# Agent attention and two MLPs in one kernel: values moving in column halves, loads reordered, running sums in a PSUM bank, the output scale moved to the end, MLP2 eight places behind

## The chip, the cores and the metric

The kernel runs on one core of a Trainium2 chip. Its time is the device time of one launch in microseconds (us); the median of three runs is the measure. The profile is one further execution. Engines are named as in the profile: PE is TensorE (matmuls; PEld is its weight load), DVE is VectorE, ACT is ScalarE, POOL is GpSimd, and SP is the engine that issues the transfers.

## The reference, cut to what matters

```python
# q, k, v: 12480 x 128; agents: 49 x 128; all float32
def sm(a, b):
    s = (a @ b.T) / sqrt(128)
    e = exp(s - s.max(-1))
    return e / (e.sum(-1) + 1e-9)
agent_v = sm(agents, k) @ v                # 49 x 128, needs every k and v
x = sm(q, agents) @ agent_v                # 12480 x 128
h = x @ w_in1                              # 128 -> 2048
g = where(h >= 1, h, where(h <= -1, 0, (h + 1)**2 / 4))
y = g @ w_out1                             # 2048 -> 128
r = maximum(y @ w_in2, 0)
out = (s * r * r + b) @ w_out2             # s and b are scalars
```

## The kernel before

Start. SP loads the keys in 12 blocks of 1,024 tokens and a rest of 192 (`KV_BLOCKS`), and puts the values block by block into the same slots once the keys there are scored. PE scores keys (`score_k`, L449), ACT copies scores out, and DVE finds maxima. The softmax over all tokens is done in two parts: blocks 0 to 5 (`EARLY`) are shifted by a first maximum, blocks 6 to 12 by the final one. The final one goes through PE twice: `turn_max(1)` (L456) and `spread_max(1)` (L463). DVE shifts a block (`shift_block`, L785), ACT takes the exponentials, DVE sums them (`sum_block`, L790), and PE multiplies values by them (`weigh_v`, L476). In `weigh_v` the 128 x 128 piece of values is the operand that is loaded as weights and the 49 exponentials, given twice (98 columns), are the one that moves. DVE then makes the transposed `agent_v_t` (L838 to L854).

Joined matrix. The kernel never forms x. `make_m` (L514) computes M = agent_v x w_in1 in five parts of 128, 384, 512, 512 and 512 columns; ACT rounds each (`round_m`), DVE makes the rest of it (`split_m`, L858), since all large matmuls run as a high and a low part. So MLP1 of a chunk is probabilities x M.

Chunks. The 12,480 tokens are 25 chunks of `W` = 500. An outer loop `i` takes chunks, an inner loop `j` has 16 places (`TILES`), one for each 128 of the 2,048 inner columns; the number n = 16 i + j is called an item here. At each place PE does, in this order: 2 matmuls of MLP1's first layer for item n (L563, L564), 3 of MLP2's first layer for an item `TILES + MLP2_DELAY` earlier (L582 to L584), 3 of MLP1's second layer for an item some places back (L545 to L547, `multiply_g1`), 3 of MLP2's second layer (L613 to L615). So a full place has 11 matmuls of 500 columns. Of the first chunk only MLP1 exists, and of the last only MLP2: from item 0 until MLP2 begins, a place has 5 matmuls. In the loop `first(i)` is chunk 0.

The first items. For n below `FIRST_ITEMS`, an item passes ACT (`below`, L694), POOL (`square_first`, L990), DVE (L886), ACT (`g1_hi`, L684), DVE (`g1_lo`, `split_g1`, L868), and then PE multiplies it (L545). Its PSUM bank is free for another item when `split_g1` is done (`h1_before`). Items below 16 rotate over five banks, all later ones over three (`h1_bank`). `second_lags` says how many places `multiply_g1` runs behind: 4 in chunk 0, 3 up to item 19, then 2.

Side jobs. Probabilities of chunk c+1 are made during chunk c: `score_q` on PE (L424, place 3), `max_q`, `shift_q`, `sum_q`, `invert_q`, `scale_q` on DVE, `exp_q` on ACT, `round_probs` and `split_probs` on POOL, `turn_probs` on PE (L432, place 12), `keep_probs` on ACT. The bias b x w_out2 summed over its rows is made by `sum_w_out2` (L526): two matmuls with one moving column at each of the places 8 to 15 of chunk 0. POOL multiplies w_out2 by s (L996) and splits it (L975, L977).

The order is the order in which each engine's code is written; engines wait for each other on semaphores. Transfers go through one queue, SP's, in program order.

## Time and profile before

| | |
|---|---|
| three runs | 1104.99, 1103.66, 1103.97 us; median 1103.97 |
| profiled execution, its own time | 1106.1 us |
| its span, first to last instruction | 1104.3 us |
| PE busy | 1088.3 us, 99% of the span |
| ACT, DVE, POOL busy | 924.3, 916.0, 843.7 us |
| PE's granted clock, mean | 0.995 of full |
| bytes read from HBM | 23.40 MB |

The page's chain that ended last is 94% PE and 3% DMA. Busy shares are means over stages that differ: in the first 47 us transfers run without a break, from 96 us on PE does. The views to look at are the tables of stretches and the order of time in the first 96 us.

### The profile page before, as it was taken

How to read it: one execution, taken by the hardware profiler on the slowest of the kernel's cores; microseconds unless marked ns; L12 is line 12 of the kernel's file. 1: busy time of each engine (PE TensorE's matmuls, PEld its weight loads, DVE VectorE, ACT ScalarE, POOL GpSimd, SP SyncE). 2: the span in 40 equal slices, each digit the busy share in tenths (PEclk: the TensorE clock that was granted, in tenths of full speed). 3: DMA queues.
4: the chain of work that ended last, by engine and by line, in shares of the span. 5: the costliest groups of instructions: out<-in, count | busy, mean ns of one | idle time of the engine just before them, and what ended most of it. 6: DMA issues, size and time to landing. Idle time of an engine off the chain costs nothing.

```text
span 1104.3 us, 16796 instructions
## 1 busy us (share of the span) xinstructions
PE 1088.3 (99%) x5349; PEld 911.3 (83%) x5349; DVE 916.0 (83%) x1456; ACT 924.3 (84%) x1745; POOL 843.7 (76%) x1231
## 2 busy tenths in 40 slices
PE   8999999999999999999999999999999999999998
PEld 7877888888888888888888888888888888888886
DVE  4677888888888888889888888888888888888876
ACT  3276888888888888888888888888888888888887
POOL 3565788788788788788788788788788788788760
PEclk9998999999999999999999999999999999999999
DMA  9700000000000000000000000000000000000000
GB/s 367 289 1 1 1 19 20 1 20 19 1 20 19 1 19 20 1 20 19 1 19 20 1 20 19 1 19 19 6 14 19 11 10 19 10 10 11 10 1 19
DMA packets 11864, 30.86 MB, mean 28 GB/s; under 512 B 1568, under 2 KB 8192, under 8 KB 11264
## 3 DMA queue, kind: packets, MB, share of 16 engines
q1 hardware_dynamic: 11776, 29.79, 7.7%
q8 instruction: 42, 0.69, 0.3%
q14 instruction: 46, 0.38, 0.1%
HBM read 23.40 MB, written 6.39 MB: 27 GB/s over the span
## 4 chain that ended last, share of the span: by engine, by line
PE 94%; DMA 3%; DVE 1%; ACT 1%; issue 0%; SPq 0%; ACTq 0%; DVEq 0%
PE ps_y L545 8%; PE ps_h L563 8%; PE ps_h L582 8%; PE ps_h L584 8%; PE ps_o L613 8%; PE ps_h L583 8%; PE ps_h L564 8%; PE ps_y L546 8%; PE ps_o L614 8%; PE ps_y L547 8%; PE ps_o L615 8%; PE ps_job L424 2%; DMA sb_kv_ring<-in_v 2%; DMA sb_kv_ring<-in_k 1%; PE ps_job L432 1%; PE ps_h L449 1%
## 5 line engine op out<-in xcount | busy, mean ns | idle before, releaser
L1022 POOL TENSOR_TENSOR sb_g_lo<-sb_square,sb_g_hi 128x500 fp32r<-128x500 f32 x380 | 484.8, 1276 | 31.7
L886 DVE SCALAR_TENSOR_TENSOR ps_h<-sb_square,ps_h 128x500 f32<-128x500 f32 (+1 forms) x400 | 272.0, 680 | 118.7 <-ACT sb_square L676 117.7
L684 ACT ACTIVATE sb_g_hi<-ps_h 128x500 fp32r<-128x500 f32 (+1 forms) x400 | 235.5, 589 | 101.3 <-DVE ps_h L886 101.3
L868 DVE SCALAR_TENSOR_TENSOR sb_g_lo<-ps_h,sb_g_hi 128x500 fp32r<-128x500 f32 (+1 forms) x400 | 270.8, 677 | 20.4 <-ACT sb_g_hi L684 11.4
L873 DVE TENSOR_SCALAR sb_below<-ps_h 128x500 f32<-128x500 f32 (+1 forms) x380 | 257.0, 676 | 11.2 <-PE ps_h L564 10.1
L705 ACT ACTIVATE sb_relu<-ps_h 128x500 f32<-128x500 f32 (+1 forms) x400 | 235.4, 589 | 24.0 <-PE ps_h L584 11.3
L714 ACT ACTIVATE sb_square<-sb_relu 128x500 f32<-128x500 f32 (+1 forms) x400 | 245.4, 614 | 0.6
L676 ACT ACTIVATE sb_square<-sb_below 128x500 f32<-128x500 f32 (+1 forms) x380 | 233.5, 615 | 0.0
L1020 POOL TENSOR_SCALAR sb_g_hi<-sb_square 128x500 fp32r<-128x500 f32 x380 | 229.1, 603 | 0.0
L1019 POOL TENSOR_TENSOR sb_gate<-sb_ones 1x1 f32<-1x1 f32 x380 | 70.5, 186 | 150.3 <-ACT sb_square L714 149.3
L545 PE MATMUL ps_y<-sb_g_hi,sb_w_out_hi 128*128 128x500 f32 (+1 forms) x400 | 160.8, 402 | 1.2 <-DVE sb_g_lo L868 1.2
L563 PE MATMUL ps_h<-sb_probs_t,sb_m_hi 113*128 113x500 f32 (+1 forms) x400 | 159.1, 398 | 2.4 <-DVE sb_g_lo L868 2.2
L613 PE MATMUL ps_o<-sb_g_hi,sb_w_out_hi 128*128 128x500 f32 (+1 forms) x400 | 155.8, 390 | 1.4 <-DVE sb_g_lo L926 0.9
L582 PE MATMUL ps_h<-sb_y_hi,sb_w_in_hi 128*128 128x500 f32 (+1 forms) x400 | 156.0, 390 | 0.2 <-DVE sb_y_lo L912 0.2
L564 PE MATMUL ps_h<-sb_probs_t,sb_m_lo 113*128 113x500 f32 (+1 forms) x400 | 156.2, 390 | 0.0
L584 PE MATMUL ps_h<-sb_y_hi,sb_w_in_lo 128*128 128x500 f32 (+1 forms) x400 | 155.9, 390 | 0.0
L546 PE MATMUL ps_y<-sb_g_hi,sb_w_out_lo 128*128 128x500 f32 (+1 forms) x400 | 155.6, 389 | 0.0
L547 PE MATMUL ps_y<-sb_g_lo,sb_w_out_hi 128*128 128x500 f32 (+1 forms) x400 | 155.2, 388 | 0.0
L615 PE MATMUL ps_o<-sb_g_lo,sb_w_out_hi 128*128 128x500 f32 (+1 forms) x400 | 155.0, 387 | 0.0
L614 PE MATMUL ps_o<-sb_g_hi,sb_w_out_lo 128*128 128x500 f32 (+1 forms) x400 | 154.9, 387 | 0.0
L583 PE MATMUL ps_h<-sb_y_lo,sb_w_in_hi 128*128 128x500 f32 (+1 forms) x400 | 154.9, 387 | 0.0
L563 PEld LDWEIGHTS ps_h<-sb_probs_t,sb_m_hi 113*128 113x128 f32 x400 | 75.6, 189 | 19.7 <-DVE sb_g_lo L868 3.1
(109 smaller groups left out, 1258.6 us busy)
## 6 DMA issues: line engine op xcount, KB each, us to landing
sb_q_ring<-in_q SPq DMA_DIRECT2D x25, 250.0 KB, 2.9
sb_kv_ring<-in_k SPq DMA_DIRECT2D x12, 512.0 KB, 9.7
sb_kv_ring<-in_v SPq DMA_DIRECT2D x12, 512.0 KB, 15.0
out<-sb_out_ring SPq DMA_DIRECT2D x24, 250.0 KB, 2.1
sb_w_stage<-in_moe_w_out SPq DMA_DIRECT2D x2, 1024.0 KB, 11.8
sb_w_stage<-in_moe_w_in SPq DMA_DIRECT2D x1, 1024.0 KB, 17.8
sb_w_in<-in_moe_w_in SPq DMA_DIRECT2D x1, 1024.0 KB, 17.6
out<-sb_out_ring SPq DMA_DIRECT2D x1, 240.0 KB, 2.0
```

What stands on the lines that cost most here:

```text
L545: pe.matmul(y_ps[:, 0:width(n)], hi, g1_hi[:, slot, 0:width(n)], start=(f == 0), stop=False)
L546: pe.matmul(y_ps[:, 0:width(n)], lo, g1_hi[:, slot, 0:width(n)], start=False, stop=False)
L563: pe.matmul(h, m_hi[:, j * 128:(j + 1) * 128], probs_t[:, phase, 0:width(n)], start=True, stop=False)
L564: pe.matmul(h, m_lo[:, j * 128:(j + 1) * 128], probs_t[:, phase, 0:width(n)], start=False, stop=True).then_inc(h1_ready, 1)
L582: pe.matmul(h, hi, y_hi[:, y_slot, 0:width(n)], start=True, stop=False)
L584: pe.matmul(h, lo, y_hi[:, y_slot, 0:width(n)], start=False, stop=True).then_inc(h2_ready, 1)
L613: pe.matmul(o_ps[:, 0:width(n)], hi, g2_hi[:, slot, 0:width(n)], start=(f == 0), stop=False)
L714: nc.scalar.activation(square2[:, place2 % WORK_RING, 0:width(n2)], relu2[:, place2 % WORK_RING, 0:width(n2)], ACT.Square).then_inc(square ...
L868: nc.vector.scalar_tensor_tensor(g1_lo[:, slot, 0:columns], h1_bank(n, place), 0.0, as_f32(g1_hi[:, slot, 0:columns]), ALU.max, ALU.subtra ...
L873: nc.vector.tensor_scalar(below[:, place % WORK_RING, 0:width(n)], h1_bank(n, place), 1.0, 1.0, ALU.min, ALU.subtract).then_inc(below_read ...
L886: nc.vector.scalar_tensor_tensor(h, square1[:, place % WORK_RING, 0:width(n)], 1.0, h, ALU.min, ALU.add).then_inc(g1_summed, 1)
L1022: nc.gpsimd.tensor_tensor(g2_lo[:, place % SPLIT_RING, 0:columns], square, as_f32(hi), ALU.subtract).then_inc(g2_split, 1)
```

## The change

What it does, by parts:

1. **Values move.** In `weigh_v` the exponentials of one tile (49 columns) are loaded as weights and the 128 value columns move. Even tiles write PSUM rows 0 to 48, odd tiles rows 64 to 112 (`half_rows`): the two column halves of PE. The sum is then 49 x 128, in two halves and two parts. ACT and DVE copy them to SBUF (`keep_values`), DVE makes a small matrix from the denominators (`a_fold`), and two matmuls (`fold_values`, L530 of the new file) give `agent_v_t`, which DVE copies once.
2. **Running sums.** `sum_block` adds the exponentials of a block, tile by tile, to a PSUM bank (392 columns); `merge_sum` reduces it once per part.
3. **Loads.** The first key block is loaded in two pieces; w_out1 goes behind all keys and q0; q1 goes behind value block 5, w_out2 behind value block 7; w_in1, in two pieces, goes behind all values.
4. **Order at the start.** `turn_max(1)` directly follows the scoring; `spread_max(1)` and then `score_q(0)` come after value block 0; `turn_probs(0)` after block 7; `score_q(1)` with `spread_sum(0)` before block 10; `turn_probs(1)` after the fold. So the side jobs of chunk 1 leave the loop of chunk 0 (`jobs`).
5. **M.** Parts 2, 3 and 4 are made at places 1, 4 and 8 (`M_STEPS`), not at 0, 1 and 2; the fourth and fifth use other banks.
6. **First items.** `FIRST_ITEMS` is 24 and all 24 rotate over five banks.
7. **MLP2** begins 8 places into chunk 1 (`MLP2_DELAY` 8, was 4). The bias sums move to the places 0 to 7 of chunk 1, with 98 moving columns. The side jobs of chunk 2 go to place 7 and 14 of chunk 1.
8. **Scale.** POOL no longer scales w_out2; ACT's output copy multiplies by s.

```diff
-MLP2_DELAY = LAG1 + 2
+MLP2_DELAY = LAG1 + 6
+J_SCORES_LATE = 7
-J_BIAS = 8
+J_TURN_P_LATE = 14
+WIDE = 98
-FIRST_ITEMS = 20
+FIRST_ITEMS = 24
...
+        first_banks = [h1_ps[0], h2_ps[0], h1_ps[1], h2_ps[1], h1_ps[2]]
...
-            if isinstance(n, int) and n < TILES:
-                return (h1_ps + h2_ps)[n % FIRST_BANKS][:, 0:W]
+            if sharing(n):
+                return first_banks[n % FIRST_BANKS][:, 0:W]
...
-        m_banks = [h2_ps[0], h2_ps[1], o_ps, y_ps, job_ps]
+        m_banks = [h2_ps[0], h2_ps[1], o_ps, job_ps, o_ps]
+        M_STEPS = [1, 4, 8]
...
-                    mm = pe.matmul(value_banks[not early(n)][:, 0:TWICE * n_agents], values, twice(a_scores[0:rows, n * KV_TILES + t], rows),
+                    mm = pe.matmul(value_banks[not early(n)][half_rows(t % 2), 0:C], a_scores[0:rows, n * KV_TILES + t], values,
...
+            def fold_values(n):
+
+                pe.wait_ge(a_fold_ready, n + 1)
+                pe.wait_ge(a_values_kept[n], 2)
+                mm = pe.matmul(h1_ps[0][:, 0:ROWS], a_values[0:ROWS, n], a_fold[0:ROWS, n, 0:ROWS], start=(n == 0), stop=(n == 1))
...
-                    mm = pe.matmul(o_ps[:, 0:1], w_stage[0][:, f * 128:(f + 1) * 128], s_b_cols[:, 1:2],
+                    mm = pe.matmul(o_ps[:, 0:WIDE], w_stage[0][:, f * 128:(f + 1) * 128], s_b_cols[:, 1:2].to_broadcast([128, WIDE]),
...
-                        nc.scalar.activation(out_ring[:, slot, 0:columns], o_ps[:, 0:columns], ACT.Identity, bias=bias_col[:]).then_inc(out_ready, 1)
+                        nc.scalar.activation(out_ring[:, slot, 0:columns], o_ps[:, 0:columns], ACT.Identity, bias=bias_col[:], scale=s_b_cols[:, 0:1]).then_inc(out_ready, 1)
...
             def sum_block(n):
...
-                nc.vector.tensor_reduce(a_sums[0:block_rows(n), n], by_agent(n), AX.X, ALU.add).then_inc(a_block_sum, 1)
+                total = sum_by_tile(not early(n))
+                if n in (0, EARLY):
+                    nc.vector.tensor_copy(total, exps(n)).then_inc(a_block_sum, 1)
+                else:
+                    dve.wait_ge(a_block_sum, n)
+                    nc.vector.tensor_tensor(total[0:rows, 0:columns], total[0:rows, 0:columns], exps(n), ALU.add).then_inc(a_block_sum, 1)
```

The queue of SP, from the transfer behind the keys to the last value. Before (in_moe_w_out is w_out1 or w_out2, in_moe_w_in is w_in2 or w_in1, in this order; the first row here is w_out1, between the sixth and the seventh key block):

```order
L379 DMA sb_w_stage<-in_moe_w_out 128x2048
L377 DMA sb_kv_ring<-in_k 128x1024 x6
L380 DMA sb_k_last<-in_k 128x192
L373 DMA sb_q_ring<-in_q 128x500
L382 DMA sb_w_stage<-in_moe_w_in 128x2048
L383 DMA sb_s_b<-in_moe_s_b 128x2
L387 DMA sb_kv_ring<-in_v 128x1024 x4
L390 DMA sb_w_stage<-in_moe_w_out 128x2048
L387 DMA sb_kv_ring<-in_v 128x1024 x4
L392 DMA sb_w_in<-in_moe_w_in 128x2048
L387 DMA sb_kv_ring<-in_v 128x1024 x4
L393 DMA sb_v_last<-in_v_last 96x256
```

After (w_out1 is the first row here, behind all keys):

```order
L418 DMA sb_w_stage<-in_moe_w_out 128x2048
L419 DMA sb_w_stage<-in_moe_w_in 128x2048
L420 DMA sb_s_b<-in_moe_s_b 128x2
L424 DMA sb_kv_ring<-in_v 128x1024 x6
L405 DMA sb_q_ring<-in_q 128x500
L424 DMA sb_kv_ring<-in_v 128x1024 x2
L429 DMA sb_w_stage<-in_moe_w_out 128x2048
L424 DMA sb_kv_ring<-in_v 128x1024 x4
L430 DMA sb_v_last<-in_v_last 96x256
L433 DMA sb_w_in<-in_moe_w_in 128x512
L434 DMA sb_w_in<-in_moe_w_in 128x1536
```

w_out1 moved behind the keys, and w_in1 moved from between the value blocks to behind them, in two pieces; one load of q and w_out2 stand between values.

PE, from value block 6 to the first matmul of M. Before:

```order
L476 MATMUL ps_o<-sb_a_scores,sb_kv_ring 128x98 x32
L432 MATMUL ps_job<-sb_ident_r,sb_probs 113x126 x4
L468 MATMUL ps_h_1<-sb_a_sum,sb_ones 128x49
L476 MATMUL ps_o<-sb_a_scores,sb_kv_ring 128x98 x16
L468 MATMUL ps_h_2<-sb_a_sum,sb_ones 128x49
L476 MATMUL ps_o<-sb_a_scores,sb_v_last 128x98 x2
L514 MATMUL ps_h_0<-sb_w_in,sb_agent_v_t 113x128
```

After:

```order
L521 MATMUL ps_o<-sb_kv_ring,sb_a_scores 49x128 x16
L476 MATMUL ps_job<-sb_ident_r,sb_probs 113x126 x4
L521 MATMUL ps_o<-sb_kv_ring,sb_a_scores 49x128 x16
L512 MATMUL ps_h_1<-sb_a_sum,sb_ones 128x49
L468 MATMUL ps_job<-sb_agents_t,sb_q_ring 126x49 x4
L521 MATMUL ps_o<-sb_kv_ring,sb_a_scores 49x128 x8
L512 MATMUL ps_h_2<-sb_a_sum,sb_ones 128x49
L521 MATMUL ps_o<-sb_kv_ring,sb_a_scores 49x128 x8
L521 MATMUL ps_o<-sb_v_last,sb_a_scores 49x128 x2
L530 MATMUL ps_h_0<-sb_a_fold,sb_a_values 128x113 x2
L476 MATMUL ps_job<-sb_ident_r,sb_probs 113x126 x4
L576 MATMUL ps_h_0<-sb_w_in,sb_agent_v_t 113x128
```

Every weighing is a matmul of 49 x 128 and no longer 128 x 98; a second `score_q` and a second `turn_probs` now stand here, and two fold matmuls.

PE, from the second matmul of M's third part (before) or the second item (after) to the first second-layer matmuls. Before:

```order
L514 MATMUL ps_o<-sb_w_in,sb_agent_v_t 113x512
L563 MATMUL ps_h_1<-sb_probs_t,sb_m_hi 128x500
L564 MATMUL ps_h_1<-sb_probs_t,sb_m_lo 128x500
L514 MATMUL ps_y<-sb_w_in,sb_agent_v_t 113x512
L563 MATMUL ps_h_2<-sb_probs_t,sb_m_hi 128x500
L564 MATMUL ps_h_2<-sb_probs_t,sb_m_lo 128x500
L514 MATMUL ps_job<-sb_w_in,sb_agent_v_t 113x512
L563 MATMUL ps_h_0<-sb_probs_t,sb_m_hi 128x500
L564 MATMUL ps_h_0<-sb_probs_t,sb_m_lo 128x500
L424 MATMUL ps_job<-sb_agents_t,sb_q_ring 126x49 x4
L563 MATMUL ps_h_1<-sb_probs_t,sb_m_hi 128x500
L564 MATMUL ps_h_1<-sb_probs_t,sb_m_lo 128x500
```

After:

```order
L624 MATMUL ps_h_0<-sb_probs_t,sb_m_hi 128x500
L625 MATMUL ps_h_0<-sb_probs_t,sb_m_lo 128x500
L576 MATMUL ps_o<-sb_w_in,sb_agent_v_t 113x512
L624 MATMUL ps_h_1<-sb_probs_t,sb_m_hi 128x500
L625 MATMUL ps_h_1<-sb_probs_t,sb_m_lo 128x500
L624 MATMUL ps_h_1<-sb_probs_t,sb_m_hi 128x500
L625 MATMUL ps_h_1<-sb_probs_t,sb_m_lo 128x500
L624 MATMUL ps_h_2<-sb_probs_t,sb_m_hi 128x500
L625 MATMUL ps_h_2<-sb_probs_t,sb_m_lo 128x500
L576 MATMUL ps_job<-sb_w_in,sb_agent_v_t 113x512
L606 MATMUL ps_y<-sb_g_hi,sb_w_out_hi 128x500
L607 MATMUL ps_y<-sb_g_hi,sb_w_out_lo 128x500
```

Between item 0 and the first multiplication there were three matmuls of M and a `score_q`; now there are two of M and no `score_q`.

## Rows read from the trace of the kernel before

**Rows 1.** Table of stretches: length, busy time of each engine, clock, DMA.

```profile
core 0: us, PE busy (x) PEld busy (x) DVE busy (x) ACT busy (x) POOL busy (x), PEclk, DMA share, GB/s
28.17:52.04 23.87, 23.81 (x207) 23.33 (x207) 16.57 (x34) 5.25 (x12) 14.65 (x7) 1.00 0.83 325
54.72:82.00 27.28, 25.32 (x119) 19.42 (x119) 20.99 (x37) 19.92 (x36) 16.54 (x18) 0.94 0.00 1
82.00:93.17 11.17, 8.76 (x33) 6.50 (x32) 7.32 (x15) 6.00 (x11) 5.00 (x5) 0.82 0.00 1
200.00:600.00 400.00, 400.00 (x1828) 334.74 (x1827) 342.36 (x537) 351.07 (x662) 325.75 (x484) 1.00 0.05 14
```

**Rows 2.** The same table, of stretches around the changes of PE's clock.

```profile
52.04:54.90 2.86, 1.30 (x6) 0.70 (x6) 1.50 (x7) 0.54 (x2) 0.00 (x0) 1.00 0.01 3
54.90:58.70 3.80, 3.80 (x9) 2.07 (x8) 1.19 (x2) 1.89 (x4) 1.02 (x1) 0.55 0.00 0
84.00:89.21 5.21, 2.81 (x10) 1.38 (x9) 3.27 (x7) 2.31 (x4) 2.53 (x3) 0.99 0.01 2
89.21:95.80 6.59, 6.59 (x20) 5.66 (x21) 4.74 (x9) 3.14 (x6) 1.02 (x1) 0.50 0.00 0
```

**Rows 3.** Order of time, 20 to 56 us: start, length, engine, line.

```profile
21.18 4.26 PE L449 MATMUL ps_h<-sb_agents_t,sb_kv_ring 128*64 128x98 f32 x96
...
27.69 0.83 DVE L775 TENSOR_REDUCE sb_a_max<-sb_a_maxes 128x49 f32<-128x392 f32 x1
...
28.17 2.03 PE L476 MATMUL ps_y<-sb_a_scores,sb_kv_ring 128*128 128x98 f32 x16 [1.38 <-DMA sb_kv_ring<-in_v]
...
32.35 7.39 PE L476 MATMUL ps_y<-sb_a_scores,sb_kv_ring 128*128 128x98 f32 x64
...
43.36 3.65 PEld L476 LDWEIGHTS ps_o<-sb_a_scores,sb_kv_ring 128*128 128x128 f32 x32 [0.23 <-DMA sb_kv_ring<-in_v]
...
53.47 1.12 PE L514 MATMUL ps_h<-sb_w_in,sb_agent_v_t 128*113 128x128 f32 x4 [1.43 <-DVE sb_agent_v_t L854]
```

**Rows 4.** Groups by line and shape, 0 to 56 us: busy, mean ns.

```profile
L785 DVE TENSOR_TENSOR sb_a_scores<-sb_a_scores,ps_h 128x392 f32<-128x392 f32 x12 | 6.7, 557 | 0.0
...
L975 POOL TENSOR_SCALAR sb_w_out_hi<-sb_w_stage 128x2048 fp32r<-128x2048 f32 x2 | 3.8, 1906 | 12.1 <-DMA sb_w_stage<-in_moe_w_out 12.0
...
L977 POOL TENSOR_TENSOR sb_w_out_lo<-sb_w_stage,sb_w_out_hi 128x2048 fp32r<-128x2048 f32 x2 | 9.1, 4552 | 0.2
```

**Rows 5.** Order of time, 56 to 84 us, PE.

```profile
61.93 1.08 PE L424 MATMUL ps_job<-sb_agents_t,sb_q_ring 128*126 128x49 f32 x8 [0.95 <-DVE sb_m_lo L858]
...
63.39 0.39 PE L545 MATMUL ps_y<-sb_g_hi,sb_w_out_hi 128*128 128x500 f32 x1
...
80.42 0.39 PE L563 MATMUL ps_h<-sb_probs_t,sb_m_hi 113*128 113x500 f32 x1
...
82.00 0.39 PE L563 MATMUL ps_h<-sb_probs_t,sb_m_hi 113*128 113x500 f32 x1
...
83.84 0.39 PE L563 MATMUL ps_h<-sb_probs_t,sb_m_hi 113*128 113x500 f32 x1
```

**Rows 6.** Order of time, 84 to 94 us, PE: items 18 and 19.

```profile
86.48 0.49 PE L563 MATMUL ps_h<-sb_probs_t,sb_m_hi 113*128 113x500 f32 x1 [0.90 <-DVE sb_g_lo L868]
...
89.21 0.78 PE L563 MATMUL ps_h<-sb_probs_t,sb_m_hi 113*128 113x500 f32 x1 [1.33 <-DVE sb_g_lo L868]
```

**Rows 7.** Groups by line, 56 to 84 us: the steps of a first item.

```profile
L990 POOL TENSOR_TENSOR sb_square<-sb_below 128x500 f32<-128x500 f32 x17 | 17.5, 1028 | 19.8 <-ACT sb_below L694 19.7
L694 ACT ACTIVATE sb_below<-ps_h,sb_half 128x500 f32<-128x500 f32 x17 | 11.5, 679 | 5.0 <-PE ps_h L564 5.0
L886 DVE SCALAR_TENSOR_TENSOR ps_h<-sb_square,ps_h 128x500 f32<-128x500 f32 x16 | 10.8, 677 | 0.0
L684 ACT ACTIVATE sb_g_hi<-ps_h 128x500 fp32r<-128x500 f32 x15 | 8.8, 584 | 0.2 <-DVE ps_h L886 0.2
```

**Rows 8.** Table of stretches, DVE alone: two pairs of its passes.

```profile
62.37:63.55 1.18, 1.18 (x4) 1.00 0.00 0
```

235 lines of the change are left out of this document (142 added, 93 removed).

## The prediction, made blind

> **What bounds the kernel now.** I read the table of stretches first, then the order of time where a stretch is not full. From 200 to 600 us PE is busy for all of 400.00 us at full clock [rows 1]. A change can shorten the middle only by taking matmuls away, and it takes none. So the time is: when MLP1 starts, how long the places with 5 matmuls take, and PE's work from there on. Three milestones cut the start of the trace before. A, the first matmul of M: 53.47 us [rows 3]. B, the first matmul of item 16: 82.00 [rows 5]. C, the first matmul of the place at which MLP2 begins (item 20): 93.17, the border of a stretch in [rows 1]. Before A the values are weighed: PE is busy for 23.81 of 23.87 us [rows 1], and 64 records of 98 columns take 7.39 us, 0.1155 each [rows 3]. Transfers are at 0.83 there, but late only by 1.38 and 0.23 us [rows 3]. Between A and B the chain of the first items rules, then a place of 1.58 us (80.42 to 82.00) [rows 5]. Between B and C PE waits 0.90 and 1.33 us for `g1_lo` [rows 6] and is busy for 8.76 of 11.17 us. Twice the clock is at half (1.2 GHz): 54.90 to 58.70, after 2.86 us with PE busy for 1.30, and 89.21 to 95.80, after 5.21 us with 2.81 busy [rows 2].
>
> **A: weighing.** A weighing record had 128 columns of weights and 98 that move; now 49 and 128, in alternate column halves. No row has this form. The nearest is the scoring: halves, 64 columns loaded, 98 move, 96 records in 4.26 us, 0.0444 each [rows 3]. With 128 moving for 98 that is 0.058. The bounds are 0.0444 and the present 0.1155. I take 0.058, since the scoring shares the alternation. A block (16 records) then takes 0.93 us, not 1.85. The Trainium skill, "TensorE: Matmul & The Clock Gate", section "Back-to-back issue gap", gives about 81 ns for each pair of weight load and matmul at 128 columns in a stream. By it a block takes 1.3 us, A comes about 1.5 us later than below, and no run here shows the form.
>
> Now transfers rule. Value block 0 lands at 28.17 as before, for the same bytes are ahead of it. From it to block 8 (43.36) 12 pieces of 0.524 MB landed (blocks 1 to 8, w_out2, w_in1; each weight is 2): 1.27 us each [rows 3]. After, 10.5 pieces lie between (w_in1 gone, half a piece of q1 more): block 8 at 41.5, 9 at 42.7, 10 at 44.0, 11 at 45.3, the rest 45.5, the first piece of w_in1 at 46.1, the second at 48.0.
>
> SP waits for w_out1's split before it issues w_out2. w_out1 now lands at about 24.3 and POOL takes 1.91 + 4.55 us [rows 4]: 30.8, while block 7 lands only at 37.7, so the queue behind does not run dry. That is free unless POOL is 4 us late.
>
> DVE is the other chain. The last maxima come some 2.3 us earlier (w_out1's two pieces, 2.5 us, no longer split the keys, and PE is then the limit), so the merge that ended at 28.52 (27.69 + 0.83 [rows 3]) ends near 26.2. But `spread_max(1)` now stands behind value block 0, which lands at 28.17: PE has little to do from 23.1 (scoring ended at 25.4) to 28.2, and the clock may fall. The late shifts start at about 30.2 (32.6 before). From there DVE has 7 shifts at 0.55 [rows 4], 11 adding passes of the same form at about 0.6 with their wait for themselves, two copies, two merges and q's passes: some 14 us, until 44.2. Before, this stretch held 16.57 us of DVE work [rows 1]; the running sum takes away about a quarter of a microsecond a block and is not on the path.
>
> PE after block 8: blocks 8 and 9 end at 43.6, sums and `score_q(1)` (1.08 [rows 5]) 44.8, block 10 45.8, block 11 and the rest 47.1. DVE has `max_q(1)` and `shift_q(1)` at 45.6, then five small passes and two for the fold to 47.5, q's three to 48.4, the copy of the values 48.7, fold 49.2, copy 49.4. POOL: w_out2 lands at 40.2, is split until 46.7, then both roundings of probabilities to 49.3, `turn_probs(1)` to 49.8. A is 49.9 with full clock. Block 8 comes after 2.9 us with almost only `turn_probs(0)`; after such gaps the clock fell twice in [rows 2]. At half clock the last part takes up to 1.5 us more. I take A = 50.4: **3.1 us earlier**. Bounds: 49.0, and 55.1 if a record stays at 0.1155 (two `score_q` and the fold are then extra).
>
> **A to B** is 28.5 us now. Three parts of M and a `score_q` that waits 0.95 us for the last part stood before the first multiplication, at 63.39, 9.9 us after A [rows 5]. After, items 0 and 1, one part, items 2 to 4, one part. With A as 0: item 0 at 1.25 as before, item 1 at 2.3, M's third part at 3.1, items 2 and 3 by 5.7 (half clock to 5.2 as before), and the chain of item 0: `below` 0.68, square 1.03, add 0.68, round 0.58, `g1_lo` 0.68 [rows 7], with M's rounding and split between: first multiplication at 7.0. Then 12 places. PE needs 5 matmuls of 0.23 (8 in 1.84 us, 82.00 to 83.84 [rows 5]), 1.15; DVE needs two passes; [rows 8] holds 1.18 us, in which two of them start (0.59 each), so 1.18 a place; ACT two, POOL 1.03. So DVE sets 1.18: 14.2, plus two splits of M of 0.6, gives 22.3. The bias matmuls (0.43 a place, 1.58 - 1.15) have left, and so has chunk 1's job. **6.2 us less.** Bounds: 21.3 (PE sets it) and 24.5 (1.3 a place and one stall of 0.6).
>
> **B to C** is now 8 places (16 to 23). PE: 16 first-layer matmuls and 27 of the second (one item extra, as the lag goes from 4 to 3), 43 at 0.23 = 9.9; 32 bias records at 0.1155, the row with 98 moving [rows 3], 3.7; `score_q(2)` 0.8; a wait of 0.7 for `g1_lo` and y's copy: 15.1, not 11.2. **3.9 us more.** But at C PE has done 4 items more, 20 matmuls: **4.6 us less** behind it. The stalls of [rows 6] go, because items 16 to 23 keep five banks: an item's trip is 3.65 us of passes and about 0.6 of matmul and hand-over, and five banks at 1.6 us give 8. The half clock after 93.17 (2.63 us at half) goes too: **1.3 us less.** Bounds of B to C: 14.2, and 18.4 with a half-clock stretch as in [rows 2].
>
> **Behind C.** For item 24 ACT and DVE change steps at full clock: 0.3 us more. The last chunk has 24 places of MLP2 alone, not 20; its matmuls are the same and PE was busy there too. The scale in ACT's output copy is in a pass that exists; POOL's multiply is gone, 2 us, off the path. Steady places: the same instructions, output copy at place 9 not 5, away from `exp_q`. Nothing.
>
> **Sum.** 3.1 + 6.2 - 3.9 + 4.6 + 1.3 - 0.3 = 11.0 us. The span of 1104.3 becomes 1093.3. The profiled execution took 1106.1 and becomes 1095.1; the median of the three runs, 1103.97, becomes **1093.0**.
>
> **Rivals.**
> - *The weighing stays bound by its weight load or by switching halves* at 0.1155: A at 55.1, 4.7 us of the gain gone, 1097.7. For it: 49-column loads still alternate with matmuls. Against: the scoring's 0.0444. 0.10.
> - *The clock falls once more*: PE waits for transfers from block 0 to 8, or DVE's 1.18 leaves PE gaps in chunk 0, and 6.6 us at half cost 3.3: 1096.3. For it: [rows 2]. Against: 1.15 of 1.18 busy. The Trainium skill, "TensorE: Matmul & The Clock Gate", section "Why this matters for your kernels", says that gaps between bursts of matmuls lower the clock; the trace agrees with 54.90 and 89.21. 0.18.
> - *A wait in every chunk.* With MLP2 at place 8, PE starts the next output sum at place 10 and waits for ACT's copy at place 9. If that copy is later than the 8 matmuls (1.8 us) between, each of 24 chunks pays; from 0.46 us a chunk the kernel is slower. With 1 us it is 1117. For it: ACT is busy for 351 of 400 us. Against: the same 8 matmuls cover it today, with no wait in [rows 1]. 0.04.
> - *The gain isn't there*: POOL's split of w_out2 holds `turn_probs(1)` and chunk 0 stalls on banks as items 16 to 19 did; all 24 places at 1.6 us: 1103. 0.04.
> - *Better than forecast*: A at 49, PE setting chunk 0: 1090.6. 0.04.
>
> **How the numbers follow.** My forecast, 1091 to 1095, has 0.60. The range 1090.3 to 1098 takes in the first two rivals and the last, 0.92, more than 0.8, since the first rival is one end of a price that no row shows; the wait in every chunk and the missing gain lie outside. A difference of 0.2% (2.2 us) is about what can be told from none. Faster 0.92, same 0.04, slower 0.04.
>
> **What would show it.** Weighing: 128 records in about 7.4 us where values are there, with waits for values at PE. A near 50.4. First multiplication 7 us behind the first matmul of M; places in chunk 0 every 1.2 us, DVE without idle time; places 16 to 23 every 1.6 us with PE full and no wait over 0.5 us; C near 88; then PE at 100%. Wrong it would be if the weighing took 1.85 us a block, if a second stretch at half clock stood between 60 and 90 us, or if PE had idle time between 200 and 600 us.

## The result, and the profile after

| | before | after |
|---|---|---|
| median | 1104.48 us (6 runs, 1102.87 to 1106.70) | 1099.14 us (6 runs, 1097.75 to 1100.54) |
| profiled execution, its span, clock | 1106.1, 1104.3, 0.995 | 1099.19, 1097.1, 0.994 |

The ratio is 0.9948, 95% interval [0.9937, 0.9959]: faster, by less than 1%. By the medians the gain is 5.3 us, about half of the 11.0 that were forecast. 1099.14 lies 1.1 us above the range. In the two traces the gain is 1104.3 - 1097.1 = 7.2 us, where the sum said 11.0.

The order of time on PE in the changed kernel up to A:

```profile
4.64 1.81 PE L493 MATMUL ps_h<-sb_agents_t,sb_kv_ring 128*64 128x98 f32 x32
8.71 1.58 PE L493 MATMUL ps_h<-sb_agents_t,sb_kv_ring 128*64 128x98 f32 x16 [2.26 <-DMA sb_kv_ring<-in_k]
...
26.14 0.58 PE L493 MATMUL ps_h<-sb_agents_t,sb_k_last 128*96 128x98 f32 x4
29.34 0.45 PE L500 MATMUL ps_job<-sb_ident,sb_a_max 128*49 128x128 f32 x1 [2.62 <-DVE sb_a_max L845]
29.72 1.95 PE L521 MATMUL ps_y<-sb_kv_ring,sb_a_scores 128*49 128x128 f32 x16
31.60 0.66 PE L507 MATMUL ps_h<-sb_ident,sb_a_tops 49*128 49x49 f32 x2
...
34.06 7.12 PE L521 MATMUL ps_y<-sb_kv_ring,sb_a_scores 128*49 128x128 f32 x80
41.01 1.91 PE L521 MATMUL ps_o<-sb_kv_ring,sb_a_scores 128*49 128x128 f32 x32
42.85 0.61 PE L476 MATMUL ps_job<-sb_ident_r,sb_probs 126*113 126x126 f32 x4
43.40 1.96 PE L521 MATMUL ps_o<-sb_kv_ring,sb_a_scores 128*49 128x128 f32 x32
...
46.51 1.08 PE L521 MATMUL ps_o<-sb_kv_ring,sb_a_scores 128*49 128x128 f32 x16
47.52 0.42 PE L512 MATMUL ps_h<-sb_a_sum,sb_ones 128*128 128x49 f32 x2
...
51.98 0.74 PE L576 MATMUL ps_h<-sb_w_in,sb_agent_v_t 128*113 128x128 f32 x3
```

The reader is to see four things. (1) A key block is 32 scoring records here. PE scores the whole first block, both of its pieces, from 4.64 on, and then waits 2.26 us for the second block. The last scores start at 26.14, where the prediction had 23.1 (25.37 before), and end at 26.72. (2) Everything behind is late with them: `turn_max(1)` at 29.34, `spread_max(1)` at 31.60. (3) 16 weighing records take 1.88 us at 29.72 (to 31.60), but 32 take 1.84 us at 41.01 (to 42.85): 0.1175 and 0.0575 us each. (4) A is 51.98, against 53.47 before [rows 3] and 50.4 forecast.

The tables of stretches of the same kernel (length, busy us of PE, PEld, DVE, ACT and POOL, PE's granted clock, DMA share, GB/s):

```profile
4.00:6.00 2.00, 2.00 (x30) 1.67 (x30) 0.00 (x0) 0.13 (x1) 0.00 (x0) 1.00 1.02 325
6.00:8.00 2.00, 0.45 (x12) 0.26 (x7) 0.25 (x1) 1.70 (x3) 0.00 (x0) 1.00 0.97 371
...
10.00:12.00 2.00, 2.00 (x28) 2.00 (x26) 0.00 (x1) 0.65 (x2) 0.00 (x0) 0.50 1.02 410
...
30.00:38.00 8.00, 8.00 (x64) 7.45 (x62) 5.53 (x14) 2.82 (x8) 7.58 (x3) 0.50 1.03 424
38.00:40.00 2.00, 2.00 (x28) 2.00 (x26) 1.97 (x7) 0.85 (x2) 0.39 (x1) 0.67 1.00 406
40.00:52.00 12.00, 10.57 (x147) 9.25 (x143) 8.20 (x23) 2.01 (x6) 8.60 (x6) 1.00 0.66 248
...
200.00:600.00 400.00, 400.00 (x1828) 334.13 (x1828) 339.87 (x535) 350.98 (x662) 326.83 (x486) 1.00 0.05 14
```

The two record prices are the two clocks: 2.4 GHz from 40 us on, half of it from 30 to 38. There are two stretches at half clock, at about 9 to 12 us and 29 to 39 us; the two of [rows 2] are gone. From 200 to 600 us PE is as full as in [rows 1].

The order of time from A on:

```profile
58.53 0.54 PE L606 MATMUL ps_y<-sb_g_hi,sb_w_out_hi 128*128 128x500 f32 x1
...
73.97 0.39 PE L624 MATMUL ps_h<-sb_probs_t,sb_m_hi 113*128 113x500 f32 x1
...
74.42 0.58 PE L589 MATMUL ps_o<-sb_s_b,sb_w_stage 128*128 128x98 f32 x4
74.78 0.47 PE L606 MATMUL ps_y<-sb_g_hi,sb_w_out_hi 128*128 128x500 f32 x1
...
81.11 0.50 PE L606 MATMUL ps_y<-sb_g_hi,sb_w_out_hi 128*128 128x500 f32 x1 [0.36 <-DVE sb_y L995]
...
82.37 0.58 PE L589 MATMUL ps_o<-sb_s_b,sb_w_stage 128*128 128x98 f32 x4
83.52 0.49 PE L606 MATMUL ps_y<-sb_g_hi,sb_w_out_hi 128*128 128x500 f32 x1 [0.57 <-DVE sb_g_lo L957]
...
90.18 0.40 PE L624 MATMUL ps_h<-sb_probs_t,sb_m_hi 113*128 113x500 f32 x1
```

The first multiplication comes 6.55 us behind A (forecast 7.0), B is 73.97 (item 16), and C, now item 24, is 90.18. Between B and C stand waits for y's copy (0.36 at 81.11) and for `g1_lo` (0.57 at 83.52). In [rows 6] it was the first layer that waited, for a bank; now it is the second layer that waits for its own `g1_lo`. These waits are longer than the brackets say, as PE's modelled ends cover the first part: where nothing is waited for, the multiplication comes 0.36 us behind the start of the four bias records (74.42 to 74.78), but 1.15 us at 82.37. What the eight places hold above 0.37 comes to 1.8 us.

| stretch | before | forecast | after |
|---|---|---|---|
| A | 53.47 | 50.4 | 51.98 |
| A to B | 28.53 | 22.3 | 21.99 |
| B to C | 11.17 | 15.1 | 16.21 |
| C to the end of the span | 1011.1 | 1005.5 | 1006.9 |
| span | 1104.3 | 1093.3 | 1097.1 |

So 3.8 us of the sum failed: 1.6 in A, 1.1 between B and C, 1.4 behind C, with 0.3 back between A and B. The forecast was made against the median of three runs, 2.1 us under the profiled execution whose trace it used. The other 0.3 us between the forecast of 1093.0 and 1099.14 is time outside the span: 2.1 us in the changed kernel, 1.8 before. The median of six executions of before is 0.5 us above that of the first three.

### The profile page after: what moved, and what is told of

Its sections match the earlier page's. It is cut to its first block, busy times and chain, and to the rows that moved or that the text cites. A ratio compares the mean times of both kernels' runs of the same rounds, so it can differ in the third digit from the quotient of the medians.

```text
span 1097.1 us, 16823 instructions
## 1 busy us (share of the span) xinstructions
PE 1081.7 (99%) x5353; PEld 901.3 (82%) x5353; DVE 910.9 (83%) x1461; ACT 926.3 (84%) x1748; POOL 839.1 (76%) x1222
## 4 chain that ended last, share of the span: by engine, by line
PE 96%; DVE 2%; ACT 1%; DMA 1%; issue 0%; POOL 0%; SPq 0%; ACTq 0%; DVEq 0%; POOLq 0%
PE ps_y L606 8%; PE ps_h L645 8%; PE ps_h L647 8%; PE ps_o L674 8%; PE ps_o L676 8%; PE ps_h L646 8%; PE ps_o L675 8%; PE ps_h L624 8%; PE ps_y L608 8%; PE ps_h L625 8%; PE ps_y L607 8%; PE ps_job L468 2%; PE ps_h L493 1%; PE ps_job L476 1%; PE ps_y L521 1%; DMA sb_kv_ring<-in_k 1%
## 5 line engine op out<-in xcount | busy, mean ns | idle before, releaser
L1104 POOL TENSOR_TENSOR sb_g_lo<-sb_square,sb_g_hi 128x500 fp32r<-128x500 f32 x376 | 479.9, 1276 | 31.3
L962 DVE TENSOR_SCALAR sb_below<-ps_h 128x500 f32<-128x500 f32 (+1 forms) x376 | 254.0, 676 | 10.0 <-PE ps_h L625 9.4
L624 PE MATMUL ps_h<-sb_probs_t,sb_m_hi 113*128 113x500 f32 (+1 forms) x400 | 156.8, 392 | 1.0 <-DVE sb_m_lo L947 0.9
L674 PEld LDWEIGHTS ps_o<-sb_g_hi,sb_w_out_hi 128*128 128x128 f32 x400 | 75.0, 188 | 19.3 <-DVE sb_g_lo L1014 4.2
```

Of the source, the lines that this page charges most:

```text
L624: pe.matmul(h, m_hi[:, j * 128:(j + 1) * 128], probs_t[:, phase, 0:width(n)], start=True, stop=False)
L674: pe.matmul(o_ps[:, 0:width(n)], hi, g2_hi[:, slot, 0:width(n)], start=(f == 0), stop=False)
L962: nc.vector.tensor_scalar(below[:, place % WORK_RING, 0:width(n)], h1_bank(n, place), 1.0, 1.0, ALU.min, ALU.subtract).then_inc(below_read ...
L1104: nc.gpsimd.tensor_tensor(g2_lo[:, place % SPLIT_RING, 0:columns], square, as_f32(hi), ALU.subtract).then_inc(g2_split, 1)
```

## The experiments

Theories, one for each stretch. For A: the split of the first key block makes scoring late, and A with it (S); its rivals are the order of the maxima (O), the landing of the keys in any case (L) or of the values (V), and VectorE's chain (D). For B to C: the lag of three items is too short (W). Behind C: the 0.05 us that a chunk takes more comes from MLP2's delay, or from the addresses. Over all of them: the clock, which falls after gaps (K). The other kernels measure a part of the change by itself. All times of A, B and C are from each kernel's order of time.

### e1_unsplit: the first key block whole

```diff
-                if n == 0:
-                    split = GROUP * 128
-                    sp.dma_start(kv_ring[:, 0, 0:split], k[:, 0:split]).then_inc(k_first_loaded, 16)
-                    sp.dma_start(kv_ring[:, 0, split:KV_COLS], k[:, split:KV_COLS]).then_inc(k_loaded[0], 16)
-                else:
-                    sp.dma_start(...)
+                sp.dma_start(kv_ring[:, n], k[:, n * KV_COLS:(n + 1) * KV_COLS]).then_inc(k_loaded[n], 16)
```

> The changed kernel, with its first key block loaded whole again. Theory S (the split costs A): in the changed kernel TensorE scored the half block at 4.64 us and then waited 2.26 us for the next key block, and the clock was at half from about 8.8 to 12 us. If the split is the cause, scoring starts near 5.1 us and runs on, the last scores end near 23 to 24 us instead of 26.7, turn_max(1) comes at 27 to 28 instead of 29.34, the half-clock stretch of 30 to 38 us shrinks, and A (first matmul of M) falls from 51.98 to 50.4 to 51.0. Time about 1.0 to 1.6 us less than the changed kernel: ratio to before 0.9934 to 0.9940. Rival O (the order rules A: spread_max(1) stands behind value block 0): scoring ends earlier but A stays within 0.3 us of 51.98, ratio 0.9948. Rival L (scoring is bound by the key blocks' landing in both): the last scores end within 0.5 us of 26.7, ratio 0.9948.

Ratio 0.9939 [0.9927, 0.9951], median 1098.54 us, profiled span 1094.3. Stretches of e1_unsplit:

```profile
4.00:6.00 2.00, 1.72 (x17) 1.35 (x17) 0.00 (x0) 0.00 (x0) 0.00 (x0) 1.00 1.01 406
6.00:8.00 2.00, 2.00 (x38) 2.00 (x36) 0.00 (x0) 1.34 (x2) 0.00 (x0) 1.00 1.03 414
...
28.00:36.00 8.00, 8.00 (x78) 7.46 (x76) 6.16 (x15) 2.82 (x7) 7.92 (x3) 0.60 1.03 423
```

and its order of time on PE:

```profile
4.99 12.03 PE L487 MATMUL ps_h<-sb_agents_t,sb_kv_ring 128*64 128x98 f32 x256 [0.28 <-DMA sb_kv_ring<-in_k]
...
23.23 0.58 PE L487 MATMUL ps_h<-sb_agents_t,sb_k_last 128*96 128x98 f32 x4
26.43 0.31 PE L494 MATMUL ps_job<-sb_ident,sb_a_max 128*49 128x128 f32 x1 [2.62 <-DVE sb_a_max L839]
...
40.27 1.08 PE L515 MATMUL ps_o<-sb_kv_ring,sb_a_scores 128*49 128x128 f32 x16 [0.57 <-DMA sb_kv_ring<-in_v]
...
49.23 1.07 PE L570 MATMUL ps_h<-sb_w_in,sb_agent_v_t 128*113 128x128 f32 x4
```

Transfers run at 406 and 414 GB/s from 4 to 8 us, against 325 and 371 in the changed kernel. 256 records are scored without a wait from 4.99 on, the last scores start at 23.23 (forecast 23.1) and end at 23.81, and A is 49.23: 2.75 us earlier than in the changed kernel, more than theory S gave. O and L fall. A to B (21.99), B to C (16.20) and what is behind C (1006.9) are those of the changed kernel to 0.01 us. But the median moves by 0.6 us only, and the intervals overlap: five of the six executions had a mean clock of 0.991 to 0.993 and spans of 1096.4 to 1097.3, the profiled one 0.996 and 1094.3. So this run alone does not show the split in the whole time.

All traces together show it at the start. In the nine whose first key block is split the rate is 219 to 325 GB/s from 4 to 6 us and 248 to 371 from 6 to 8; in the eight without the split it is 404 to 416 and 399 to 418. A repeats only to about 1 us, even where nothing ahead of it differs (51.98 in the changed kernel, 51.42 in e3_lag4, 52.33 in e4_wide1). Still, it is 51.42 to 53.02 in the six kernels with the split and the loads and weighing of the change, and 49.23 to 50.27 in five of the six without the split; the sixth, e2_spread, has 52.77 with a stretch at half clock, shown below.

The rate is not the whole of it. By an estimate from the two tables 0.25 MB are missing at 8 us, which is 0.6 us of the queue, but PE has to wait 2.26 us. The second key block landed 6.6 us after its issue in the changed kernel and 4.5 us in e1_unsplit. Why it comes so late, and why the rate falls, no run shows.

### e7_split_before: the split alone, in the kernel before

```diff
-                sp.dma_start(kv_ring[:, n], k[:, n * KV_COLS:(n + 1) * KV_COLS]).then_inc(k_loaded[n], 16)
+                if n == 0:
+                    split = GROUP * 128
+                    sp.dma_start(kv_ring[:, 0, 0:split], k[:, 0:split]).then_inc(k_first_loaded, 16)
+                    ...
```

> The kernel before, with the first key block loaded in two pieces as in the changed kernel, and nothing else. Theory S: TensorE starts on the half block at 4.6 us, waits some 2.3 us for key block 1, and the last scores end 2 to 3 us later than the 25.9 us of before, at 28 to 28.5. Value block 0 lands at 28.2 and from there TensorE was full for 23.8 us, so most of the delay falls into the time in which it waited anyway: A (53.47) comes 0.3 to 1.0 us later; ratio to before 1.000 to 1.001, and a half-clock stretch between 8 and 12 us may show. Rival (the late start of scoring in the changed kernel came from something else, the load of q or w_out1): the last scores end within 0.5 us of 25.9 here.

Ratio 1.0012 [1.0003, 1.0020]. Stretches of e7_split_before:

```profile
4.00:6.00 2.00, 2.00 (x34) 1.67 (x34) 0.00 (x0) 0.28 (x1) 0.00 (x0) 1.00 0.91 240
6.00:8.00 2.00, 0.29 (x8) 0.10 (x4) 0.33 (x1) 1.55 (x3) 0.00 (x0) 1.00 0.88 293
```

and its order of time on PE:

```profile
8.82 6.96 PE L455 MATMUL ps_h<-sb_agents_t,sb_kv_ring 128*64 128x98 f32 x160 [2.52 <-DMA sb_kv_ring<-in_k]
...
55.74 1.79 PE L520 MATMUL ps_h<-sb_w_in,sb_agent_v_t 128*113 128x128 f32 x4 [1.44 <-DVE sb_agent_v_t L860]
```

The same loss in a kernel with nothing else changed: 240 and 293 GB/s from 4 to 8 us, a wait of 2.52 us for the second key block, scores until 29.2, and A at 55.74. That is 2.3 us behind [rows 3] and 1.2 behind e5_before_delay8 (54.52), whose start is also that of before. 0.3 to 1.0 us was expected: the slack in front of the weighing took up less of the delay. The split by itself costs 1.3 us of the median, and the interval lies just clear of 1.

### e9_loads: the loads in the order of before

```diff
+                if n == EARLY - 1:
+                    sp.dma_start(w_stage[0][:], w_out1).then_inc(w_out1_loaded, 16)
...
-                if n == 7:
+                if n == 3:
                     sp.wait_ge(w_out1_split, 1)
                     sp.dma_start(w_stage[0][:], w_out2).then_inc(w_out2_loaded, 16)
+                if n == 7:
+                    ...   # the two pieces of w_in1, which stood behind all values
```

> The changed kernel with the loads in the order of before: w_out1 between the keys (behind the sixth key block), w_out2 behind value block 3, w_in1 (in its two pieces) behind value block 7 instead of at the end. Theory R (the order of the loads is worth something, as A hangs on the last values): the keys' last blocks land 2.5 us later, the last scores end at 27.5 to 28.5 and not 26.7, value blocks 8 to 11 come 2.5 us later as w_in1 stands ahead of them, and A moves from 51.98 to 53.5 to 54.5: ratio to before 0.996 to 0.9975. Rival (A hangs on VectorE and TensorE alone): A within 0.5 us of 51.98, ratio 0.9948.

Ratio 0.9976 [0.9964, 0.9988]; scores end at 28.47, A is 53.32, 1.34 us behind the changed kernel's. The interval lies clear of the changed kernel's, so the order of the loads is worth something: by the two ratios 3 us, by the two traces 1.3, of which up to 1 us may be the spread of A. The clocks of its executions are 0.989 to 0.996, so a part may be the clock's.

### e6_halves: the same weighing without alternate halves

```diff
-  mm = pe.matmul(value_banks[not early(n)][half_rows(t % 2), 0:C], a_scores[0:rows, n * KV_TILES + t], values,
+  mm = pe.matmul(value_banks[not early(n)][half_rows(int(t == block_tiles(n) - 1)), 0:C], a_scores[0:rows, n * KV_TILES + t], values,
```

> The changed kernel, in which the 15 first value tiles of a block all go to one column half and only the last to the other: the same 49 columns of weights and 128 that move in each record, without the alternation. Theory H (the alternation lets one record's weights load while the other runs): a record takes 0.11 to 0.12 us at full clock instead of 0.0575, the weighing of 196 records grows by some 10 us, TensorE and not DVE sets A, and A moves from 51.98 to 55 to 58; ratio to before 0.998 to 1.001. Rival F (49 columns of weights are a small enough load by themselves): the records stay at 0.06 to 0.065 us, A within 0.3 us of 51.98, ratio 0.9948.

Ratio 0.9989 [0.9979, 1.0000]. The order of time of e6_halves, in a stretch with a granted clock of 1.00:

```profile
49.10 1.73 PE L521 MATMUL ps_o<-sb_kv_ring,sb_a_scores 128*49 128x128 f32 x16
50.76 0.42 PE L512 MATMUL ps_h<-sb_a_sum,sb_ones 128*128 128x49 f32 x2
...
55.23 1.06 PE L576 MATMUL ps_h<-sb_w_in,sb_agent_v_t 128*113 128x128 f32 x4
```

16 records take 1.66 us (49.10 to 50.76), 0.104 each, against 1.01 us (46.51 to 47.52) in the changed kernel. The shape is the same, 49 columns loaded and 128 moving; the alternation alone makes the difference. A is 55.23 and the median 1103.85 us, against 1105.00 for before. Without it nearly all of the gain of the change is gone. The Trainium skill, "TensorE: Matmul & The Clock Gate", section "Back-to-back issue gap", gives some 81 ns (0.081 us) for each pair of weight load and matmul at 128 columns in a stream: the traces have 0.063 us with alternate halves and 0.104 without, one on either side of it.

### e3_lag4: four items behind, for items 16 to 23

```diff
-            if n == TILES:
-                return [LAG_FIRST, LAG1 + 1]
             if n < FIRST_ITEMS:
-                return [LAG1 + 1]
-            return [LAG1 + 1, LAG1] if n == FIRST_ITEMS else [LAG1]
+                return [LAG_FIRST]
+            return [LAG_FIRST, LAG1 + 1, LAG1] if n == FIRST_ITEMS else [LAG1]
...
-            return LAG1 if isinstance(i, int) and i == 1 else LAG1 - 1
+            return LAG1 + 1 if isinstance(i, int) and i == 1 else LAG1 - 1
```

> The changed kernel, with the second multiplication four items behind (not three) for items 16 to 23, and the copy of y one place later. Theory W (the lag of three leaves too little time for g1_lo on the way from B to C): the waits of 1.4 us for g1_lo and 0.36 us for y's copy in this stretch fall to under 0.5 us together, C (90.18 us) comes 1.0 to 1.3 us earlier, at about 89.0, less 0.7 us as one multiplication of three matmuls moves behind C, and the whole is 1 us shorter: ratio to before about 0.9938. Rival: DVE sets the pace of these places at any lag (it has its two passes an item and the copies), so the waits move behind item 23 or into waits for banks, C plus what lies behind it stays the same within 0.3 us, ratio 0.9948.

Ratio 0.9938 [0.9926, 0.9950]. The order of time of e3_lag4 (the wait stands in brackets):

```profile
81.25 0.58 PE L587 MATMUL ps_o<-sb_s_b,sb_w_stage 128*128 128x98 f32 x4
82.44 0.50 PE L604 MATMUL ps_y<-sb_g_hi,sb_w_out_hi 128*128 128x500 f32 x1 [0.60 <-DVE sb_y L993]
...
88.85 0.39 PE L622 MATMUL ps_h<-sb_probs_t,sb_m_hi 113*128 113x500 f32 x1
```

B to C takes 14.36 us (74.49 to 88.85) instead of 16.21; one wait is left, 0.60 us for y's copy, and none for `g1_lo`. What the eight places hold above 0.37 falls from 1.8 to 0.8 us. 0.7 us more is the one multiplication of three matmuls that moved behind C. There it costs only 0.2 us (1007.1), for in the changed kernel PE waited for `g1_lo` behind C as well (0.20 us at 92.37). Net 1.65 us, more than the 1 us expected: theory W holds, and three items were too few. A to B had a stretch at half clock here and took 23.07, which hides most of it in this trace.

### e4_wide1: bias sums with one moving column

```diff
-WIDE = 98
+WIDE = 1
```

> The changed kernel, with bias sums of 1 moving column instead of 98. In the trace of the changed kernel four bias records with 98 columns take 0.53 us a place (84.75 to 85.28), in that of before four with 1 column 0.37. Theory N (the width does nothing but cost): 8 places shorten by 0.16 us, but only where TensorE is the last; since it waits for g1_lo in these places, 0 to 1.3 us are won, and I expect 0.3: ratio to before 0.9935 to 0.9948, clock at full throughout B to C. Rival K (the width keeps the clock): with 1 column TensorE does less in these places, waits more for g1_lo, and the granted clock falls to half within 74 to 100 us for 3 to 7 us, which costs 1 to 3 us: ratio 0.9957 to 0.9975.

Ratio 0.9960 [0.9944, 0.9976], from 12 executions. B to C takes 16.19 us, as with 98 columns (16.21). My expectation misread a row: the 0.53 us of a place (84.75 to 85.28) held a wait; with 1 column it is 0.53 there too (86.01 to 86.54 in e4_wide1), and without a wait four records with 98 columns take 0.36 (74.42 in the changed kernel), four with 1 column 0.37 in before. The granted clock was 1.00 from 76 to 100 us. So the width costs nothing in the trace, and in the profiled execution kept no clock either. The interval overlaps that of the changed kernel. Two of the 12 executions had a clock of 0.987 and spans of 1103.1 and 1104.3; where they lost it no trace shows, so theory K is neither shown nor excluded for them.

### e5_before_delay8: MLP2 eight places in, in the kernel before

```diff
-MLP2_DELAY = LAG1 + 2
+MLP2_DELAY = LAG1 + 6
```

> The kernel before, with MLP2 eight places in and not four, and nothing else. A chunk took 41.155 us in the trace of before and 41.207 in that of the changed kernel, without an idle time of TensorE. Theory D (the delay changes what meets in a place, and this costs 0.05 us a chunk): a chunk takes 41.20 to 41.21 us. Rival: another part of the change does it, and a chunk stays at 41.155. For the whole: items 20 to 23 now go through three banks without MLP2's matmuls in between, each with a wait of 0.9 to 1.3 us as at 86.48 and 89.21 in [rows 6], and nothing on TensorE is saved by the delay, so 3 to 5 us slower: ratio to before 1.003 to 1.0045. If the five banks were not needed for those places, it is within 0.1% of before.

Ratio 1.0017 [1.0008, 1.0026]. A chunk takes 41.154 us ((975.04 - 110.81) / 21, from `turn_probs` to `turn_probs`): the delay isn't what costs 0.05 us. The whole is slower, as expected, but by 1.9 us (by the ratio) and not by 3 to 5. Where the five banks are missing, the wait of [rows 6] comes once more, at item 20, and behind it the second layer waits for its own `g1_lo`:

```profile
91.62 0.50 PE L563 MATMUL ps_h<-sb_probs_t,sb_m_hi 113*128 113x500 f32 x1 [0.72 <-DVE sb_g_lo L868]
...
94.23 0.49 PE L545 MATMUL ps_y<-sb_g_hi,sb_w_out_hi 128*128 128x500 f32 x1 [1.22 <-DVE sb_g_lo L868]
```

### e11_pad: the addresses of before

```diff
+        a_sums = sb("a_sums", [128, BLOCKS, n_agents])
         a_sum = sb("a_sum", [128, 2, n_agents])
...
-        a_values = sb("a_values", [ROWS, 2, C])
-        ...
+        a_part = sb("a_part", [128, n_agents])
+        a_rest = sb("a_rest", [128, n_agents])
...
         out_ring = sb("out_ring", [128, IO_RING, W])
+        a_values = sb("a_values", [ROWS, 2, C])
+        ...
```

> The changed kernel, with every large tensor at the address that it has in the kernel before: the small tensors of before (a_sums, a_part, a_rest) are allocated again, unused, and a_values, halves and a_fold stand at the end. No instruction changes. A chunk took 41.155 us in the traces of before, e5_before_delay8 and e7_split_before, and 41.205 in the changed kernel, e1_unsplit, e3_lag4 and e4_wide1, spread over all matmuls. Theory A (the addresses of the operands that move, probs_t, g_hi, g_lo and y_hi, decide it): a chunk takes 41.15 to 41.16 us, and the whole is 1.2 us shorter. Rival (another difference in every chunk, such as the scale that ScalarE applies to the output, or where the instructions lie): 41.20 to 41.21, and ratio to before 0.9948.

`turn_probs` of the same two chunks, 20 chunks apart, in the changed kernel and then in e11_pad:

```profile
142.59 0.52 PE L476 MATMUL ps_job<-sb_ident_r,sb_probs 126*113 126x126 f32 x4
...
966.69 0.52 PE L476 MATMUL ps_job<-sb_ident_r,sb_probs 126*113 126x126 f32 x4
```

```profile
143.35 0.52 PE L479 MATMUL ps_job<-sb_ident_r,sb_probs 126*113 126x126 f32 x4
...
966.41 0.52 PE L479 MATMUL ps_job<-sb_ident_r,sb_probs 126*113 126x126 f32 x4
```

(966.69 - 142.59) / 20 = 41.205, (966.41 - 143.35) / 20 = 41.153. No instruction differs, only where tensors lie. The same holds over all traces: a chunk takes 41.15 us in before, e5_before_delay8, e7_split_before, e11_pad and e13_final, and 41.20 to 41.21 in the twelve others, whatever else was changed in them. C to the end is 1005.7 us, where the prediction said 1005.5 and the changed kernel had 1006.9. Theory A holds. The ratio of this kernel alone, 0.9946 [0.9934, 0.9958], doesn't show it, since A was later in its trace (52.80) and its clocks lay between 0.992 and 0.997. In whole times no pair of runs shows it clear of noise.

### e14_pad8 and e15_pad56: which property of the address

```diff
+        pad = sb("pad", [128, 2])      # [128, 14] in e15_pad56
         q_ring = sb("q_ring", [C, IO_RING, W])
```

> The changed kernel with an unused tensor of 8 bytes a partition ahead of q_ring, and nothing else: probs_t, y_hi, g_hi and g_lo move by 8 bytes, or by a whole unit if tensors are placed on a grid. The small tensors of before that are gone add up to 696 bytes more than the new ones, which is 8 above a multiple of 16. Theory 16: what counts is where an operand lies within 16 bytes, and a chunk takes 41.15 to 41.16 us here and with 56 bytes. Theory 64: it counts where it lies within 64 bytes: 41.205 or another value here, 41.155 with 56 bytes. Rival (something else about the place): 41.205 in both.

> The changed kernel with an unused tensor of 56 bytes a partition ahead of q_ring. Theory 16 and theory 64: a chunk takes 41.15 to 41.16 us, since 56 bytes bring each tensor to where it lies in the kernel before, within 64 bytes. Rival: 41.205.

(966.62 - 142.52) / 20 and (969.02 - 144.79) / 20 are 41.205 and 41.212: the small shifts change nothing in the mean, though single chunks went from 41.14 to 41.29 (in the changed kernel they repeat 41.22, 41.16, 41.24). Theories 16 and 64 fall. Each kernel ran once: 1099.17 and 1101.47 us.

e14_pad8 shows one thing more. Its start is that of the changed kernel but for the addresses, and there PE did wait for value block 8:

```profile
42.87 1.08 PE L522 MATMUL ps_o<-sb_kv_ring,sb_a_scores 128*49 128x128 f32 x16 [0.62 <-DMA sb_kv_ring<-in_v]
```

That is 2.6 us later than in e1_unsplit (40.27), and A is 51.86. So the split does not only delay the scores: the values land later too.

### e2_spread and e10_awake: the order of the maxima, and filled gaps

e2_spread is e1_unsplit with

```diff
             turn_max(1)
+            spread_max(1)
+            pe.wait_ge(a_top_ready, 2)
+            score_q(0, 0, 0)
             for n in range(BLOCKS):
-                if n == 1:
-                    ...
```

> The kernel of e1_unsplit, with spread_max(1) and score_q(0) directly behind turn_max(1), ahead of the first value block. In e1_unsplit turn_max(1) came at 26.43 us, TensorE then waited 0.55 us for value block 0, weighed it at half clock, and spread_max(1) came at 28.86; the clock was at half from 28 to 35 us, and in five of its six executions the mean clock was lower still (0.991 to 0.993, against 0.996 in the profiled one). Theory V (A is set by the landing of the last values, and by the chain behind them): spread_max(1) comes at about 26.9, 2 us earlier, the late shifts too, but A stays at 49.2, within 0.3 us. Rival D (VectorE's shifts and sums set A): A falls by 1 to 2 us, to 47.5 to 48.2. For the clock: if the small work fills the gap in front of the first value block, the half clock stretch is shorter or gone and the median of the executions falls by 1 to 2 us, ratio to before 0.992 to 0.993; if not, 0.9935 to 0.994.

and e10_awake is e1_unsplit with

```diff
+            keep_awake(14)
             turn_max(1)
+            keep_awake(3)
...
                     turn_probs(0)
+                    keep_awake(10, h1_ps[0])
```

> The kernel of e1_unsplit with filling work for TensorE, whose result nobody reads: 14 transposes of the identity ahead of turn_max(1) and 3 behind it (ahead of value block 0), and 10 behind turn_probs(0) (ahead of value block 8). Thirteen of them took 2.1 us at the start of the program. In e1_unsplit the clock was at half from 28 to 35 us, after 24 to 28 us with TensorE busy for 1.02 of 4.00 us; in e2_spread at half from 43 to 55 us, after 38 to 40 us with TensorE busy for 0.62 of 2.00. Theory K (the half clock comes from these gaps, and differs from one execution to the next since some gaps lie near the edge): with the gaps filled the clock is full from 24 to 46 us, A stays at 49.2 to 49.6 (the values' landing sets it), and the executions agree: mean clock 0.998 or more in each, spans 1093.5 to 1094.5, ratio to before 0.990 to 0.9915. Rival (the clock falls for reasons outside these gaps): clocks of 0.991 to 0.996 and ratio 0.9935 to 0.994 as e1_unsplit.

e2_spread: ratio 0.9938 [0.9924, 0.9952], profiled span 1098.8 with a clock of 0.991. Stretches there:

```profile
38.00:40.00 2.00, 0.62 (x6) 0.47 (x4) 1.69 (x4) 0.64 (x2) 0.83 (x2) 1.00 1.02 418
...
44.00:52.00 8.00, 7.93 (x52) 6.73 (x52) 3.26 (x13) 0.63 (x2) 3.22 (x3) 0.50 0.37 136
```

and the order of time on PE:

```profile
40.62 2.97 PE L515 MATMUL ps_o<-sb_kv_ring,sb_a_scores 128*49 128x128 f32 x32 [1.62 <-DMA sb_kv_ring<-in_v]
...
52.77 1.99 PE L568 MATMUL ps_h<-sb_w_in,sb_agent_v_t 128*113 128x128 f32 x4
```

`spread_max(1)` came 1.3 us earlier (27.52), PE had weighed 8 blocks by 38 us, waited 1.62 us for value block 8, and the clock was at half from about 42 to 56: A at 52.77. This shows where an execution with a clock of 0.991 loses its time. e8_best, with the same start, has A at 49.69.

e10_awake: ratio 0.9933 [0.9921, 0.9945]. Stretches there, and the same of e1_unsplit in the second fence:

```profile
28.00:36.00 8.00, 7.10 (x110) 6.30 (x106) 7.08 (x18) 3.35 (x8) 7.92 (x3) 1.00 1.03 420
50.00:58.00 8.00, 7.79 (x17) 4.29 (x16) 4.15 (x8) 5.22 (x11) 3.75 (x4) 0.57 0.00 0
```

```profile
50.00:58.00 8.00, 6.95 (x25) 4.23 (x24) 5.67 (x11) 6.91 (x15) 5.06 (x5) 1.00 0.00 1
```

The filling did what it was to do from 24 to 50 us (clock 1.00), and A came at 49.33, as in e1_unsplit, where 28 to 36 us had a clock of 0.60. So the half clock there does not set A; both kernels wait for value block 8, until 40.27 and 40.39, and have the same work behind it. Nor does VectorE: in e2_spread its last full shift started 1.9 us earlier than in e1_unsplit (33.76 against 35.69), and PE still waited for value block 8 until 40.62. Theory V holds for the kernels without the split, D falls. The executions of e10_awake have clocks of 0.996 to 0.999, against mostly 0.991 to 0.993 in e1_unsplit, but the two ratios overlap. But the clock then fell from 50 to 58 us (0.57), and A to B took 23.80 instead of 21.99. Theory K named the wrong gaps: 46 to 50 us, the end of the sums and the fold, with PE busy for 2.56 of 4.00 us, was not filled. In e1_unsplit the same stretch was followed by full clock; why it is so in one execution and not in the next no run here shows.

### e8_best, e12_all, e13_final: the parts together

e8_best is e2_spread with the lag of e3_lag4; e12_all adds the filling of e10_awake; e13_final adds the addresses of e11_pad.

> The kernel of e2_spread (key block whole, spread_max(1) and score_q(0) ahead of value block 0) with the lag of four of e3_lag4. e3_lag4 won 1.85 us between B and C and gave 0.2 back behind C. Theory W again: B to C takes 14.4 us and not 16.2, C to the end 1007.1, so that the median is 1.6 us under that of e2_spread (1097.62), near 1096.0: ratio to before 0.992. Rival: the gain depends on where the clock stands, and the median is within 0.5 us of e2_spread's.

> The kernel of e8_best with the filling transposes of e10_awake (14 ahead of turn_max(1), 3 behind it, 10 ahead of value block 8). Theory K and theory V (the landing of the last values sets A): A at 49.0 to 49.5, B to C 14.4, no stretch at half clock from 24 to 90 us, spans 1091.8 to 1092.8, median 1094 to 1095, ratio to before 0.9905 to 0.991. If VectorE's shifts and sums set A (rival D), spread_max(1) two us earlier brings A to 47.5 to 48.2 and the median to 1093. If the clock falls in spite of the filling, the median is that of e8_best.

> The kernel of e12_all (ratio 0.9918) with the tensors at the addresses that they have in the kernel before, as in e11_pad. If the parts add up, a chunk takes 41.153 us and not 41.205, C to the end 1005.9 and not 1007.1, and the median is 1.2 us lower, near 1094.8: ratio to before 0.9905 to 0.991. Rival (the clock between 46 and 60 us differs so much from one execution to the next that it hides this): the profile shows 1.2 us less behind C, and the median is within 0.5 us of 1096.0.

| | ratio | median us | A | A to B | B to C | C to end | clocks |
|---|---|---|---|---|---|---|---|
| changed kernel | 0.9948 [0.9937, 0.9959] | 1099.14 | 51.98 | 21.99 | 16.21 | 1006.9 | 0.991 to 0.996 |
| e8_best | 0.9936 [0.9923, 0.9948] | 1098.30 | 49.69 | 22.91 | 14.39 | 1007.1 | 0.992 to 0.997 |
| e12_all | 0.9918 [0.9905, 0.9931] | 1096.00 | 49.35 | 24.00 | 14.39 | 1007.1 | 0.995 to 1.000 |
| e13_final | 0.9905 [0.9889, 0.9922] | 1094.77 | 50.27 | 23.18 | 14.34 | 1006.0 | 0.996 to 1.000 |

e8_best missed its forecast of 1096.0: its executions run from 1095.0 us (clock 0.997) to 1099.4 (0.992). With the filling they run from 1095.0 to 1097.5, and e12_all's median is 2.3 us lower; it came out 1 us above its forecast, as the clock still fell behind A (A to B 24.00). e13_final took off another 1.2 us of the median, as expected, and 1.1 us behind C, though the intervals of the two ratios overlap. It is the fastest: 10.4 us under the 1105.19 of before measured beside it. That is near the 11.0 of the prediction's sum, but by other means: the split, the lag and the addresses are mended, `spread_max(1)` comes earlier, and gaps are filled.

## Where the prediction was right, and where it failed

**Weighing, right.** 0.058 us a record was taken, 0.0575 to 0.063 measured at full clock; e6_halves shows that it hangs on the alternation.

**A, wrong by 1.6 us.** The step that failed is "The last maxima come some 2.3 us earlier". They came 0.8 us later: `turn_max(1)`, which waits for them, starts at 29.34, and the merge of before ended at 28.52. The prediction never priced the split of the first key block; it counted bytes of the queue, not the rate at which they come in the first microseconds, nor how late the next block lands. e1_unsplit and e7_split_before show the split as the cause from both sides: 2.75 us of A in the one, 1.2 to 2.3 in the other. It also fails "Value block 0 lands at 28.17 as before": with the split it lands at 29.01 in e3_lag4 and 29.95 in e4_wide1, without it at 27.29 in e1_unsplit. Without the split the last scores started 0.1 us from the forecast, and A was 1.2 us better than it, as value block 8 landed at 40.27 and not at 41.5. So the sum had two errors here, and the smaller hid a part of the larger. The half clock, of which the prediction's "the clock may fall" spoke, came from 29 to 39 us. Without the split it is hidden, as PE waits for value block 8 anyhow (e10_awake). What it costs where the split is, no run separates.

**A to B, right** (21.99 for 22.3): first multiplication at 6.55 for 7.0, and the pace of 12 places behind it.

**B to C, mis-sized by 1.1 us.** The term was "a wait of 0.7"; the first-layer stalls of [rows 6] did go, but waits for `g1_lo` and for y's copy of 1.8 us in all stand behind the bias records. Two other terms missed and cancelled, which was luck: the 32 bias records take 3.0 us (0.37 a place) and not 3.7, and the 43 matmuls some 0.7 us more than 9.9, as the first matmul behind bias records or a wait takes 0.31 to 0.33 us and not 0.23. With a lag of four the stretch is 14.36 us, below the forecast. The bias records' 98 columns were no part of it (e4_wide1).

**Behind C, wrong by 1.4 us.** The step is "Steady places: the same instructions ... Nothing." The instructions are the same, and a chunk took 0.05 us more, 1.2 us in 24 chunks, with no idle time to see. e11_pad shows that the addresses did it: with those of before, C to the end is 1005.7 us, 0.2 from the forecast. The first suspect, MLP2's delay, was cleared by e5_before_delay8.

**The level, 2.1 us (and 0.3 outside the span).** The gain was taken from the median of three runs, while the trace it was worked out on was of an execution 2.1 us longer. Executions of before lie on levels: spans of 1101.0 at a clock of 1.000, 1103.5 at 0.995. The change takes away two half-clock stretches of [rows 2] and brings two of its own, so what a median gains is not what the cleaner trace gains. The rival "the clock falls once more" was right in that the clock fell, but not on how. It expected waits for transfers from block 0 to 8 or gaps in chunk 0. The half clock came behind the wait for the second key block and behind 2.62 us of waiting for the maxima. From 52 to 100 us the clock was full. Its 1096.3 is no hit: the split, the lag and the addresses account for the terms that failed.

## What to carry to other kernels

Price a split transfer by what it does to the rate at the start of a saturated queue, and ask what comes right behind the piece that lands early: an engine that starts sooner and then waits may end later, and lose its clock too. Where an engine is full for a microsecond count that matters, look at the time of one trip of the loop to a hundredth, before and after: identical instructions can run at another pace when unrelated small tensors move the large ones. And compare a forecast to several executions with their clocks, not to one trace: here A moved by 1 us between traces in which nothing ahead of it differed.

## What the runs showed of the hardware

- Two transfers of 256 KB in place of one of 512 KB at the head of the queue lowered the rate to 219 to 325 GB/s from 4 to 6 us and 248 to 371 from 6 to 8 us (nine traces), from 404 to 416 and 399 to 418 (eight traces). The loss is not made up: summed over its stretches, e7_split_before had moved 14.67 MB by 40 us, and before 15.24. PE began on the second key block at 7.4 to 9.1 us with the split. Why, is open.
- 49 weight columns and 128 that move: 0.0575 to 0.063 us a record in alternate column halves, 0.104 in the same half.
- The place of the operands in SBUF moved the pace of full-clock matmuls by 0.13% (41.205 against 41.153 us a chunk), with another value for each of three chunks in turn. Shifts by 8 and 56 bytes changed the three values and not their mean; which property of the address counts is open.
- The clock of one and the same program differs between executions: 0.991 to 0.996 for the changed kernel, with spans of 1095.7 to 1098.4 us. With filling transposes in the gaps ahead of A it was 0.996 to 0.999 (e10_awake), but the half clock still came behind A.
